# Layer 1 in two tiles of 256 tokens and five of 512, with two chunks of attention in the prologue in place of three

## What is computed

```python
# 4 batches, 8 heads, 768 steps, head size 48
for t in range(S):
    state = alpha[:, :, t, :, None] * state + einsum('bhd,bhe->bhde', k[:, :, t], v[:, :, t])
    y[:, :, t] = einsum('bhd,bhde->bhe', q[:, :, t], state)
x = y.transpose(0, 2, 1, 3).reshape(3072, 384)
x = (sigmoid(x @ w_gate) * (x @ w_val)) @ w_out            # layer 1, width 1536
x = maximum(maximum(x @ w1, x @ w2), x @ w3) @ w_out2      # layer 2, width 768
```

## Time and profile before

| what | value |
|---|---|
| median of 3 runs | 843.97 us |
| the profiled execution, its own time | 843.96 us |
| its span in the profile | 842.2 us |
| TensorE matmuls busy | 834.4 us, 99% |
| weight loads busy | 731.6 us, 87% |
| VectorE busy | 384.4 us, 46% |
| ScalarE busy | 274.6 us, 33% |
| GpSimd busy | 74.4 us, 9% |

### The profile page before, as it was taken

How to read it: one execution, slowest core, us unless ns; L and a number is a source line. 1 busy time by engine, 2 the same in 40 slices (tenths; PEclk the granted TensorE clock), 3 DMA queues, 4 the chain that set the end, 5 groups by cost and what they waited for, 6 DMA issues and landing times.

```text
span 842.2 us, 15966 instructions
## 1 busy us (share of the span) xinstructions
PE 834.4 (99%) x6673; PEld 731.6 (87%) x6673; DVE 384.4 (46%) x932; ACT 274.6 (33%) x490; POOL 74.4 (9%) x68
## 2 busy tenths in 40 slices
PE   8999999999999999999999999999999999999998
PEld 7899999999999988788878888888888888888887
DVE  8787455556567656554653322323223232222321
ACT  4655333333334433334232343322213122121312
POOL 1000111111112101110210044100000000000000
PEclk9999999999999999999999999999999999999999
DMA  7441111111112211210112022000101001010101
GB/s 289 159 188 49 54 49 48 55 49 49 54 48 75 79 34 37 74 57 4 46 49 85 1 75 75 1 1 1 38 0 38 0 0 37 0 37 0 37 1 38
DMA packets 14271, 42.35 MB, mean 50 GB/s; under 512 B 1888, under 2 KB 5472, under 8 KB 14208
## 3 DMA queue, kind: packets, MB, share of 16 engines
q1 hardware_dynamic: 14144, 41.41, 14.0%
q10 hardware_dynamic: 64, 0.05, 0.0%
HBM read 35.56 MB, written 4.72 MB: 48 GB/s over the span
## 4 chain that ended last, share of the span: by engine, by line
PE 97%; DVE 2%; DMA 1%; issue 1%; ACT 0%; SPq 0%; DVEq 0%
PE ps_gv L1039 35%; PE ps_out L1063 19%; PE ps_gv L1045 18%; PE ps_out L1155 6%; PE ps_sc L1039 6%; PE ps_sc L1045 3%; PE ps_pair L1155 2%; PE ps_pair L1013 1%; PE ps_pair L995 1%; PE ps_pair L946 1%; PE ps_sc L966 1%; PE ps_sc L980 1%; PE ps_pair L966 0%; DVE rdec L714 0%; DVE decay L699 0%
## 5 line engine op out<-in xcount | busy, mean ns | idle before, releaser
L1039 PE MATMUL ps_gv<-x_hi,w_hi 128*128 128x512 f32 (+1 forms) x720 | 267.1, 371 | 1.1 <-ACT x_hi L473 1.1
L1039 PE MATMUL ps_gv<-x_hi,w_lo 128*128 128x512 f32 (+1 forms) x720 | 264.7, 368 | 0.0
L1045 PE MATMUL ps_gv<-x_lo,w_hi 128*128 128x512 f32 (+1 forms) x720 | 226.2, 368 | 0.0
L1039 PEld LDWEIGHTS ps_gv<-x_hi,w_hi 128*128 128x128 f32 x720 | 135.2, 188 | 17.4 <-ACT w_hi L473 1.3
L1045 PEld LDWEIGHTS ps_gv<-x_lo,w_hi 128*128 128x128 f32 x720 | 133.8, 188 | 17.9
L1039 PEld LDWEIGHTS ps_gv<-x_hi,w_lo 128*128 128x128 f32 x720 | 135.3, 188 | 15.7
L813 DVE TENSOR_TENSOR h_sb<-act_sb,ps_gv 128x384 f32<-128x384 f32 (+1 forms) x84 | 51.2, 610 | 149.2 <-PE ps_gv L1045 149.2
L473 ACT ACTIVATE h_hi<-h_sb 128x384 fp32r<-128x384 f32 (+1 forms) x84 | 48.0, 571 | 146.5 <-DVE h_sb L813 146.1
L517 ACT ACTIVATE act_sb<-ps_gv 128x384 f32<-128x384 f32 (+1 forms) x84 | 45.1, 537 | 142.4 <-PE ps_gv L1045 142.4
L910 DVE TENSOR_TENSOR probs<-probs,ps_gv 128x512 f32<-128x512 f32 x36 | 24.7, 687 | 138.4 <-PE ps_gv L1045 138.4
L777 DVE TENSOR_TENSOR h_lo<-h_sb,h_hi 128x384 fp32r<-128x384 f32 (+1 forms) x84 | 51.7, 615 | 49.1 <-ACT h_hi L473 49.1
(11 more groups left out here) (128 smaller groups left out, 971.2 us busy)
## 6 DMA issues: line engine op xcount, KB each, us to landing
inbuf<-att_in SPq DMA_DIRECT2D x23, 704.0 KB, 4.6
mid<-w SPq DMA_DIRECT2D x12, 576.0 KB, 7.7
inbuf<-att_in SPq DMA_DIRECT2D x23, 256.0 KB, 2.8
inbuf<-w SPq DMA_DIRECT2D x6, 768.0 KB, 4.4
out<-inbuf SPq DMA_DIRECT2D x5, 768.0 KB, 3.5
out<-inbuf SPq DMA_DIRECT2D x4, 192.0 KB, 2.0
mid<-att_in SPq DMA_DIRECT2D x1, 704.0 KB, 8.4
x_raw<-x_raw SPq DMA_DIRECT2D x18, 32.0 KB, 2.0
```

Source lines behind the costliest of these rows:

```text
L1039: mm(bank, w_at(half, f, c + k * P, total=total), x_hi[:, k, 0:w], start=(k == 0 and half == 0), stop=False)
L1045: return mm(bank, w_at(0, f, c + k * P, total=total), x_lo[:, k, 0:w], start=False, stop=(k == KT - 1))
```

## The change

- `SIZES` is (256, 256, 512, 512, 512, 512, 512); `PRO`, the number of chunks in the prologue, falls from 3 to 2, and so chunks 2 and 3 are scored in tile 0 and chunks 4 to 7 in tile 1.
- New step lists: `TWO` for tile 0 (scores in 3 and 8), `TIGHT` for tile 1. The inverse scans have steps of their own (`recip`).
- In tiles 0 and 1 VectorE runs `scans` behind h_lo and new_state, not ahead of the masks. In tile 0 its weight blocks are split in thirds: one third beside h_hi (between h_sb and h_lo), two thirds behind h_lo, or all of it, or scans, by `beside_h_hi` and `behind_h_lo`.
- `crossed` begins at chunk 8 (`FIRST[3]`) in place of chunk 6.
- Chunk 1's y has banks of its own, chunk 2 an ordinary buffer. The outer products of chunk 1 come in step 0 of tile 0, and new_state(1) there too.
- The prologue is in another order on every engine; SP loads four weight blocks early and chunk 3 behind the eighth.

```diff
-SIZES = (384, 384, 384, 384, 512, 512, 512)
+SIZES = (256, 256, 512, 512, 512, 512, 512)
...
-THREE = {"scan": (0, 3, 6), "score": (2, 5, 8), "add": (4, 7, 9)}
-FOUR = {"scan": (-2, 2, 4, 6), "score": (1, 4, 6, 8), "add": (3, 5, 7, 9)}
-STEPS = (THREE, THREE, THREE, FOUR, FOUR, FOUR)
+TWO = {"scan": (), "recip": (), "score": (3, 8), "add": ()}
+TIGHT = {"scan": (-2, 0, 3, 6), "recip": (-2, 1, 4, 6), "score": (1, 4, 6, 8), "add": ()}
+FOUR = {"scan": (-2, 2, 4, 6), "recip": (-2, 2, 4, 6), "score": (1, 4, 6, 8), "add": (3, 5, 7, 9)}
+STEPS = (TWO, TIGHT, FOUR, FOUR, FOUR, FOUR)
+CROSSED = FIRST[3]
...
# SP
-            load_chunk(2)
-            for f in range(1, RING - 3):
+            for f in range(1, 4):
                 load_w1(f)
-            load_alpha(3)
+            load_alpha(2)
             move_last(0, (0, 2))
-            load_qkv(3)
-            load_chunk(4)
-            for f in range(RING - 3, NF1):
+            load_qkv(2)
+            for f in range(4, RING):
                 load_w1(f)
-            load_chunk(5)
+            load_chunk(3)
+            for f in range(RING, NF1):
+                load_w1(f)
...
# ScalarE, prologue
+            act.wait_ge(consts_in, 16)
+            check(0)
             khs_copy(0)
             split_w1(0)
-            act.wait_ge(consts_in, 16)
-            khs_copy(1)
+            split_w1(1)
+            split_w1(2)
             y_copy(0)
-            split_w1(1)
-            check(0)
-            distance(1)
-            khs_copy(2)
-            violation(1)
             y_copy(1)
-            y_copy(2)
...
-            split_w1(2)
+            khs_copy(1)
...
# ScalarE, tile 0, behind h_hi and what follows it
                     split_w1(f + 3)
                     if f == 1:
-                        check(2)
+                        check(1)
...
# VectorE, tile 0
+            def beside_h_hi(f):
+                if f == 0:
+                    recips(2, (0,))
+                elif f in (2, 7):
+                    scale_q(2 if f == 2 else 3)
+                elif f == 6:
+                    recips(3, (0, 1))
+                elif f <= 9:
+                    split_w1(f + 2, (0,))
+            def behind_h_lo(f):
+                if f == 0:
+                    new_state(1)
+                    recips(2, (1, 2, 3))
+                elif f in (2, 7):
+                    scale_k(2 if f == 2 else 3)
+                    split_w1(f + 2)
+                elif f == 6:
+                    split_w1(8)
+                    recips(3, (2, 3))
+                elif f <= 9 and f not in (3, 8):
+                    split_w1(f + 2, (1, 2))
+                if f == 4:
+                    scans(3)
...
-                    if scanned is not None:
+                    if scanned is not None and T > 1:
                         scans(scanned)
...
+                    elif T == 0:
+                        beside_h_hi(f)
                     h_rest(f, h_hi_done, h_lo_done, g, h_sb[:, 0:w], w)
+                    if T == 0:
+                        behind_h_lo(f)
                     if scored is not None:
                         new_state(scored)
-                    if scanned is not None:
-                        recips(scanned, range(PAIRS))
+                    if scanned is not None and T <= 1:
+                        scans(scanned)
+                    if inverted is not None:
+                        recips(inverted, range(PAIRS))
                     if added is not None and crossed(added):
                         y_add(added)
-                    if T == 0 and f in (0, 4, 7):
-                        scale_qk(PRO + (0, 4, 7).index(f))
-                    if T == 0 and f + 2 < NF1:
-                        split_w1(f + 2)
+                    if T == 0 and f in (3, 8):
+                        split_w1(f + 2, (1, 2))
...
# TensorE, prologue and step 0
             scores(1)
+            attend(0)
+            attend(1)
             transposes(1)
-            attend(0)
-            outer(1)
-            unused(10, ident, ident)
-            scores(2)
-            transposes(2)
-            attend(1)
-            outer(2)
-            attend(2)
-            unused(12, ident, ident)
+            unused(7, ident, ident)
...
                     product(ps_val[:, 0:w], f, DM, W1C).then_inc(val_done, 1)
+                    if g == 0:
+                        outer(1)
```

More of the change, by code:

```diff
@@ L123, in build @@
         stage_in = [sem(f"stage_in{n}") for n in range(RING)]
-        att_loaded = [sem(f"att_loaded{b}") for b in range(3)]
+        att_loaded = [sem(f"att_loaded{b}") for b in range(2)]
         state_zero, zeros_done, rend_done = (sem(n) for n in ("state_zero", "zeros_done", "rend_done"))
-        alpha_loaded = [sem(f"alpha_loaded{b}") for b in range(3)]
+        alpha_loaded = [sem(f"alpha_loaded{b}") for b in range(2)]
         w_hi_done, w_lo_done = sem("w_hi_done"), sem("w_lo_done")
@@ L158, in buf @@
         def buf(C):
-            return 2 if C == 2 else C % 2
+            return C % 2
         def buf_cols(b, lo, n, rows=slice(0, P)):
-            if b == 2:
-                lo += (RING - 2) * W1C
-                return mid[rows, lo:lo + n]
             return inbuf[rows, b * INC + lo:b * INC + lo + n]
@@ L206, in y_banks @@
         def y_banks(C):
-            two = ps_gv if C == 1 else ps_pair
+            two = ps_out[:, 1:KT, :].rearrange("p k c -> p (k c)") if C == 1 else ps_pair
             return two[:, 512 - 2 * CH:512 + 2 * CH].rearrange("p (s t) -> p s t", s=PAIRS)
         def crossed(C):
-            return C >= FIRST[2]
+            return C >= CROSSED
         def cross_bank(s):
@@ L257, in arrived @@
         def arrived(eng, sems, C):
[L259 to L264, removed]
+            eng.wait_ge(sems[C % 2], (C // 2 + 1) * 16)
         w_slow, w2_slow = inbuf[:, 0:W1C], inbuf[:, INC:INC + W2C]
@@ L303, in load_alpha @@
                 b, a = buf(C), PAIRS * CH
[L304 to L307, removed]
+                if C >= 2:
                     sp.wait_ge(y_done, C - 1)
@@ L722, in masked @@
                 if half == 0 and not (C < 2):
-                    dve.wait_ge(y_done, 3 if C == 3 else C - 1)
+                    dve.wait_ge(y_done, C - 1)
                 n, w = subs(C), CH // subs(C)
@@ L783, in split_w1, with scale_q, scale_k @@
                 dve.wait_ge(w_lo_done, f)
[L784 to L788, removed]
+                lo, hi = parts[0] * DM, (parts[-1] + 1) * DM
+                a = slice(f * W1C + lo, f * W1C + hi)
+                ins = nc.vector.tensor_tensor(w_lo[:, a], slot(f)[:, lo:hi], w_hi[:, a].bitcast(F32), ALU.subtract)
+                if hi == W1C:
+                    ins.then_inc(w_lo_done, 1)
+            def scale_q(C):
                 arrived(dve, att_loaded, C)
                 dve.wait_ge(scan_done, scans_by(C))
-                q, k = att(buf(C), Q), att(buf(C), K)
+                q = att(buf(C), Q)
                 nc.vector.tensor_tensor(q, q, decay[0:PR, C % 2], ALU.mult).then_inc(qh_done, 1)
+            def scale_k(C):
                 dve.wait_ge(rdec_done, scans_by(C))
+                k = att(buf(C), K)
                 nc.vector.tensor_tensor(k, k, rdec[0:PR], ALU.mult).then_inc(kh_done, 2)
+            def beside_h_hi(f):
[21 more added lines that the diff above has]
+                    scans(3)
             def layer1(T, hooks):
@@ L801, in layer1 @@
                     g = T * NF1 + f
-                    scanned, scored, added = (chunk_at(T, f, steps) for steps in ("scan", "score", "add"))
-                    if scanned == PRO:
-                        scanned = None
-                    if scanned is not None:
+                    scanned, inverted, scored, added = (
+                        chunk_at(T, f, what) for what in ("scan", "recip", "score", "add"))
+                    if scanned is not None and T > 1:
                         scans(scanned)
@@ L866, in _ @@
             recips(0, range(PAIRS))
-            scale_qk(0)
+            scale_q(0)
+            scale_k(0)
             scans(1)
             recips(1, range(PAIRS))
-            scale_qk(1)
+            scale_q(1)
+            scale_k(1)
             dve.wait_ge(consts_in, 16)
@@ L875, in _ @@
             new_state(0)
-            scans(2)
-            recips(2, range(PAIRS))
-            scale_qk(2)
             masked(1, 0)
             masked(1, 1)
-            masked(2, 0)
-            masked(2, 1)
-            new_state(1)
-            new_state(2)
             split_w1(1)
-            scans(3)
+            split_w1(2)
+            scans(2)
             for k in range(KT):
                 x_rest(k, k, x_of(0, k))
-            recips(3, range(PAIRS))
             def sum_violations():
@@ L1116, in unused @@
                 for _ in range(n):
[L1117 removed]
+                    mm(ps_out[:, 0, 0:CH], left, right, start=True, stop=True)
             zeros = state[:, 0, :, :].rearrange("p a e -> p (a e)")
```

26 lines of the change are left out of this document (10 added, 16 removed).

## The result

The changed kernel takes 857.13 us (median of 4 runs, 855.72 to 858.59), the kernel before 843.98 beside it; the ratio is 1.0157, 95% interval 1.0144 to 1.0169. It is slower, as forecast, by 13.15 us where 4.1 were forecast, and outside the range (842.0 to 851.5). Its four runs lie 1.4 us apart, and the mean granted clock goes with them: 855.72 us at 0.996, 857.13 and 857.14 at 0.994, 858.59 at 0.992. These are the means that two, three and four stretches of 3.41 us at half clock give; the profile, at 857.13, has three. The kernel before stands at 1.0 within 0.2 us.

The account below looks back on a forecast made before the run. TensorE, with 97% of the chain, was taken as the bound. Start of layer 1 (-7.8), TensorE work (+5.1) and stalls (+6.8) summed to +4.1 us, giving 848.1 us; range 842.0 to 851.5.

Parts of the forecast that it names:

- 1, start of layer 1: Prologue: first `val` product starts at 21.8 us in place of 29.63, -7.8 us.
- 2, TensorE work: TensorE work after layer 1 starts: more left to do, mostly uncrossed attention, with passes of 256 at 120 ns; +5.1 us.
- (a): Tile 0, steps 1 to 3: gate(3) waits 0.4 us behind a late sigmoid, scores of chunk 2 wait 0.9; together 1.3.
- (b): Tile 0, step 8: VectorE comes late to h_sb(7), so scores of chunk 3 wait 0.85 us.
- (c): Tile 0 to 1: VectorE's scans in step 10 delay h_sb(11) and x_hi; 1.85 plus 0.5 for GpSimd, together 2.3 us.
- (d): Tile 1 to 2: the same step 10, with chunk 8 and tokens of 512 behind it; 1.8 + 0.5 = 2.3 us.
- step 8 of tile 1: Rest of tile 1: attention covers the scans, waits of 0.2 us at most, counted as nothing.
- R4: Rival: weight loads bind, so passes of 256 columns are no shorter than now; +34 us, 878; chance 0.03.
- Term 3: Stalls of TensorE in and between tiles 0, 1 and 2: +6.8 us, ends 2 and 9.
- R3: Rival: the array's clock falls before layer 1, behind a gap of 1.6 us; 3 us more, 851; chance 0.05.

Follow-up runs that it names:

- experiment 1: Changed kernel with unused matmuls filling TensorE's three long waits, nothing else changed: 853.02 us, ratio 1.0109 to the kernel before.
- experiment 6: On top of experiment 5, ScalarE checks chunk 1 in step 2 of tile 0 in place of step 1: 846.63 us, ratio 1.0028.
- experiment 7: On top of experiment 6, inverse scans of chunks 3, 4 and 8 spread over two steps each: 843.33 us, ratio 0.9998.
- experiment 3: Changed kernel with the scans of chunks 4 and 8 one step earlier, in step 9 of the tile before: 849.55 us, ratio 1.0072.
- experiment 9: Kernel before (tiles of 384) with useless VectorE multiplications behind h_lo in step 10 of tiles 0 and 1: 849.75 us, ratio 1.0068.
- experiment 2: Changed kernel with GpSimd scaling q of chunks 4, 7 and 8 only after VectorE's eight inverse scans: 856.28 us, ratio 1.0153.
- experiment 4: Changed kernel with the scans of chunk 7 ahead of the masks in step 6 of tile 1: 855.20 us, ratio 1.013.
- experiment 5: Changed kernel with the changes of experiment 3 and experiment 4 together: 847.57 us, ratio 1.0041.
- experiment 8: On top of experiment 7, 12 unused matmuls in place of 7 fill the gap ahead of layer 1: 843.29 us (11 runs), ratio 0.9993.

## Why the prediction was wrong, by its own steps

| term | forecast | measured | from |
|---|---|---|---|
| 1, start of layer 1 | -7.8 | -7.6 | first `val` at 22.01 for 29.63 |
| 2, TensorE work | +5.1 | +4.3 | what is left in experiment 1, from the first `val` to the first product of layer 2's output (539.2 us for 523.7), less the five waits below |
| (a) steps 2 and 3 of tile 0 | 1.3 | 1.26 | 0.38 + 0.88 |
| (b) step 8 of tile 0 | 0.85 | 0.92 | gate to scores 2.09 for 1.17 |
| (c) tile 0 to 1 | 2.3 | 3.4 | experiment 1 |
| (d) tile 1 to 2 | 2.3 | 3.4 | experiment 1 |
| step 8 of tile 1 | 0 | 2.3 | experiment 1 |
| half clock | 0 | 4.1 | changed kernel less experiment 1 |
| end of the program | 0 | +0.9 | last matmul to end, 3.93 for 3.00 |
| sum | +4.1 | +13.0 | of 13.15 by the runs |

**What held.** The start came at 22.0 us where 21.8 were said. A pass of 256 columns comes 0.12 us after the last (68.34, 68.46 in the rows above): the straight line through 384 and 512 holds, and R4 is out; weight loads were no floor. Step (a) held to its parts: the sigmoid behind the check was to start 8.05 us after the first `val`, and it starts 8.10 behind it, at 30.11:

```profile
30.02 0.19 ACT L575 ACTIVATION_READ_ACCUMULATOR inbuf<-inbuf,cst 128x1 f32 x1
30.11 0.36 ACT L505 ACTIVATE act_sb<-ps_gv 128x256 f32<-128x256 f32 x1
```

Experiments 6 and 7 took (a) and (b) away where the prediction placed them; 3 and 9 show (c)'s chain in both kernels. The sign and the mechanism of the waits were right. Term 3, the stalls, was not: 6.8 us were forecast, with 9 as its end, and the waits are 11.3, with 4.1 of half clock behind them. That TensorE's work came 0.8 us lower than forecast, and nearly makes up for the end of the program, is luck; where the 0.8 come from is open.

**Where it failed.** First, in (c) and (d), "While GpSimd scales q the eight rdec scans take 2.52 in place of 2.03; from chunk 4 on it does, at that moment: +0.5." The row was misread. In it GpSimd's multiply of q is over before the inverse scans start at 289.28, and what lies beside them is one multiply of k, half as long:

```profile
286.68 1.29 POOL L441 TENSOR_TENSOR inbuf<-inbuf,decay 112x512 f32<-112x512 f32 x1 [16.44 <-DVE decay L699]
...
290.43 0.74 POOL L445 TENSOR_TENSOR inbuf<-inbuf,rdec 112x256 f32<-112x256 f32 x1 [2.46 <-DVE rdec L714]
```

In a step that has scans and inverse scans together q and k both lie beside them, and they last 3.38 (2.03 with GpSimd held back, experiment 2). That is 0.9 of the 1.1 us that are missing at either end of tile 1. Second, "In tile 1 otherwise recips and scans stand in steps with attention beside them, ... and I find waits of 0.2 at most": chunk 7 has scans, inverse scans and new_state in one step, and h_sb(7) comes over 3 us late, as h_sb(11) does. What TensorE needs behind it is then not x_hi but ScalarE's copy of chunk 6's y, and the scores come 2.3 us late. Third, and most: the waits were priced as waits alone. The prediction had the clock only as R3, for the prologue, at 0.05. The Trainium skill ("TensorE: Matmul & The Clock Gate", Part 1) says that idle time brings the array back to half rate; the trace agrees, and the rule should have been put to every hole that the sum itself made, not to one: 2 to 3 us of standing still cost 1.4 us more, three times over. R3 itself came true in some executions (experiments 4 to 7), at 1.4 us and not at 3.

The upper end of the range, 851.5, took in passes of 125 ns or one fall of the clock, each by itself; longer waits with a fall behind each of three lay outside it.

Without waits of its own the plan is worth little. Experiment 8 is the change with its stalls removed: 843.29 us, 0.6 under the kernel before and not separable from it by its interval. Taking the third chunk out of the prologue gives 7.6 us there; of these 5.6 come back between the first `val` and layer 2 (529.3 us for 523.7) and 1.2 behind the last matmul (4.15 for 3.00).

## What to carry to other kernels

Narrowing a tile shortens TensorE's step, and leaves work that doesn't go by tokens, like the scans, as long as it was. List for each other engine the longest such block that it runs behind its last due operation, and compare it with the new step, above all where a tile ends and the next one's operands wait behind it. Then follow what each engine does next: here a copy two operations further on held TensorE up. Where a profile says "issue", take the kernel's waits one by one and see which ended last. Price a new wait of TensorE in two parts, the wait and the half clock behind it, and if the wait can't go, fill it with unused matmuls (4.1 us here). Take the duration of an operation that another engine slows from a row in which the other is busy beside it for as long as it will be.

## What was not expected of the hardware

- The half clock doesn't follow a hole of a given length each time. Behind the gap of 1.6 us in the prologue it came in four of eleven executions of experiment 7. One of 2.2 us, at the scores of chunk 7, brought it in the profile of the changed kernel and not in that of experiment 3, and the two of 3.1 us did in the changed kernel. The hole of 2.72 us in experiment 9 was followed by none in the profile. Each stretch recorded was 3.41 us long, and each cost about 1.4 us.
- Eight inverse scans last 2.03 us with none of GpSimd's multiplies beside them, 2.52 with 0.7 us of them (the kernel before, experiment 3) and 3.39 with 1.8; three x_lo last 1.62 or 3.20.
